# Eight heads' global scores in one block a batch, and eight value tiles a head instead of nine

## The reference, cut to what matters

```python
# 4 batches, 8 heads, 512 local and 32 global tokens, head size 64
k_all = concatenate([k_g, k_l]); v_all = concatenate([v_g, v_l])       # 544 keys
out_g = softmax(scale * q_g @ k_all.T) @ v_all                         # the 32 global queries see all
s_ll  = where(|i - j| <= 32, scale * q_l @ k_l.T, -1e9)                # local ones see a window of 32
out_l = softmax([scale * q_l @ k_g.T, s_ll]) @ v_all                   # and the global keys
x = [out_g, out_l] as 2304 tokens x 512
x = soft mixture of 8 experts (router phi, w1, relu, w2) of x
out = (h - tanh(h)) @ w_out,  h = x @ w_in
```

## Time and profile before

| | us |
|---|---|
| median of 3 runs (lowest, highest) | 318.64 (318.07, 319.13) |
| time of the profiled execution | 318.87 |
| its span | 317.1 |
| busy: PE, DVE, ACT, POOL | 306.9, 211.9, 139.0, 64.8 |

### The profile page before, as it was taken

How to read it: one execution, slowest core, us unless ns; L and a number is a source line. 1 busy time by engine, 2 the same in 40 slices (tenths; PEclk the granted TensorE clock), 3 DMA queues, 4 the chain that set the end, 5 groups by cost and what they waited for, 6 DMA issues and landing times.

```text
span 317.1 us, 7840 instructions
## 1 busy us (share of the span) xinstructions
PE 306.9 (97%) x2987; PEld 220.3 (69%) x2987; DVE 211.9 (67%) x443; ACT 139.0 (44%) x293; POOL 64.8 (20%) x62
## 2 busy tenths in 40 slices
PE   7999999999999999999998999999999999999994
PEld 4576777777777786233335888788888888888883
DVE  3887988888889556721258877566556666566572
ACT  1366766666566642111137554432334222532531
POOL 0543434434335001000008964000000000000000
PEclk9999999999999999999999999999999999999999
DMA  7999999999999969999999000030003000300202
GB/s 236 376 375 341 334 377 407 370 401 372 375 390 343 391 232 378 414 407 412 415 419 406 21 2 0 1 132 2 0 0 134 0 0 0 135 1 0 99 2 74
DMA packets 18032, 69.56 MB, mean 219 GB/s; under 512 B 4176, under 2 KB 5840, under 8 KB 14288
## 3 DMA queue, kind: packets, MB, share of 16 engines
q1 hardware_dynamic: 18000, 69.14, 57.7%
HBM read 64.41 MB, written 4.46 MB: 217 GB/s over the span
## 4 chain that ended last, share of the span: by engine, by line
PE 86%; DVE 7%; issue 5%; ACT 1%; POOL 1%; DVEq 0%; POOLq 0%
PE ps L846 20%; PE ps L849 20%; PE ps L550 6%; PE ps L595 5%; PE ps L821 5%; PE ps L746 4%; PE ps L777 4%; PE ps L587 3%; PE ps L566 3%; DVE sc L1101 3%; PE ps L606 2%; PE ps L541 2%; PE ps L560 2%; PE ps L581 2%; PE ps L658 1%
## 5 line engine op out<-in xcount | busy, mean ns | idle before, releaser
L849 PE MATMUL ps<-wlo,gg 128*128 128x512 f32 x204 | 80.5, 395 | 0.0
L846 PE MATMUL ps<-whi,gg 128*128 128x512 f32 x204 | 80.3, 394 | 0.0
L1307 DVE SCALAR_TENSOR_TENSOR nt<-uu,ps 128x512 f32<-128x512 f32 (+2 forms) x80 | 48.4, 607 | 47.3 <-ACT uu L1008 47.1
L1008 ACT ACTIVATE uu<-ps 128x512 f32<-128x512 f32 (+2 forms) x80 | 42.8, 537 | 84.0 <-PE ps L821 78.2
L457 POOL TENSOR_TENSOR sc<-sc,mx 128x640 f32<-128x640 f32 x32 | 40.1, 1253 | 53.5 <-DVE mx L1106 53.5
L1318 DVE TENSOR_TENSOR gg<-nt,ps 128x512 fp32r<-128x512 f32 (+2 forms) x80 | 47.9, 601 | 0.1
L846 PEld LDWEIGHTS ps<-whi,gg 128*128 128x128 f32 x204 | 38.4, 188 | 8.8
L849 PEld LDWEIGHTS ps<-wlo,gg 128*128 128x128 f32 x204 | 38.4, 188 | 8.0
L1101 DVE TENSOR_TENSOR sc<-ps,cst 128x640 f32<-128x640 f32 x32 | 26.2, 820 | 7.5 <-PE ps L550 5.9
L821 PE MATMUL ps<-cT,Pst 128*128 128x512 f32 (+2 forms) x80 | 28.9, 361 | 0.7 <-DVE Pst L1289 0.6
L595 PEld LDWEIGHTS ps<-vv,eT 128*64 128x64 f32 x512 | 18.7, 137 | 13.4 <-issue 11.0
(11 more groups left out here) (130 smaller groups left out, 384.6 us busy)
## 6 DMA issues: line engine op xcount, KB each, us to landing
w<-moe_w SPq DMA_DIRECT2D x11, 2048.0 KB, 11.2
vv<-v_t SPq DMA_DIRECT2D x8, 1170.0 KB, 7.7
w<-moe_w SPq DMA_DIRECT2D x14, 512.0 KB, 11.6
kT<-k_t SPq DMA_DIRECT2D x16, 416.0 KB, 6.3
out<-oo SPq DMA_DIRECT2D x17, 256.0 KB, 2.2
qT<-q_t SPq DMA_DIRECT2D x16, 256.0 KB, 7.3
win<-moe_w_in SPq DMA_DIRECT2D x4, 1024.0 KB, 16.6
wout<-moe_w_out SPq DMA_DIRECT2D x3, 1024.0 KB, 22.2
```

Of the source, the lines that this page charges most:

```text
L846: pe.matmul(o, g, hi, start=(c == 0), stop=False)
L849: mm = pe.matmul(o, g, lo, start=False, stop=(c == NC - 1))
L1008: nc.scalar.activation(uu[c % 2][:, 0:width], cols(h_bank(i, c), width), ACT.Square, scale=(1.0 / 3) ** 0.5).then_inc(square_ready, 1)
L1307: nc.vector.scalar_tensor_tensor(out=nt[c % 2][:, 0:width], in0=uu[c % 2][:, 0:width], scalar=1.0, in1=cols(h_bank(i, c), width), op0=ALU. ...
```

## The change

The scores of both global units of a batch are made in one block, `scores(4)`: eight matmuls of 512 keys, then two times four of 32 keys. Unit 4 uses banks 0 and 1, unit 9 banks 2 and 3. Head j of unit 9 puts its 32 queries at rows `32 * (j ^ 1)` instead of `32 * j`, so that heads j and j+4, which read the same 64 rows, write other columns. `SCORES_AT` loses unit 9, so at k=4 no scores are made. `rank` gives the new order of the score counters (0 to 4, 9, 5 to 8). DVE passes both global units after `normalise` of unit 9 (`global_maxima`) and nothing after that of unit 4; `scg` and `gmx` are there twice.

A global unit's last 32 keys are now transposed as the end of a block of 96 columns, so they land on rows 64 to 95 of `eT`, and are weighed with those rows of the last odd value tile, by matmuls of 32 rows, second in the order of the tiles. The fifth even tile is gone from the layout and from the loads (1040 KB a load instead of 1170).

The loads of the last two pairs' keys and of the global queries count on one semaphore, and they, and the queries, are issued in another order.

```diff
-        SCORES_AT = {(u - AHEAD) % U: u for u in (0, 2, 4, 5, 7, 9)}
+        SCORES_AT = {(u - AHEAD) % U: u for u in (0, 2, 4, 5, 7)}
+        GR = P // 2 + SG
+        def rank(k):
+            return k if k < 5 else 5 if k == 9 else k + 1
+        def global_rows(qd, j):
+            return 32 * (j ^ qd)
-            return 0 if k in GQ else 2 * head_of(k)[1]
+            return 2 * (k // 5) if k in GQ else 2 * head_of(k)[1]
...
             def keys(i, pr):
-                sp.wait_ge(scores_ready, U * (i - 1) + GQ[pr // 2] + 1)
+                sp.wait_ge(scores_ready, U * (i - 1) + (6, 6, 8, 10)[pr])
...
             global_queries(1)
+            keys(1, 2)
+            keys(1, 3)
             sp.wait_ge(zeros_ready, 2)
             values(1, 0)
-            keys(1, 2)
             queries(1, 2)
-            keys(1, 3)
             queries(1, 3)
...
                 queries(i + 1, 0)
                 queries(i + 1, 1)
+                global_queries(i + 1)
+                keys(i + 1, 2)
+                queries(i + 1, 2)
                 load_w1(sp, i - 1, w1_loaded, w1s[i - 1][:])
-                keys(i + 1, 2)
                 keys(i + 1, 3)
-                global_queries(i + 1)
+                queries(i + 1, 3)
                 values(i + 1, 0)
-                queries(i + 1, 2)
-                queries(i + 1, 3)
...
                 if k in GQ:
-                    pe.wait_ge(qg_loaded, 16 * i)
-                    pe.wait_ge(masked_ready, U * i + k - 1)
+                    pe.wait_ge(global_loaded, 48 * i)
                 else:
...
+                pe.wait_ge(masked_ready, U * i + rank(k))
...
+                    for j in range(4):
+                        for qd in range(2):
+                            one(qd, j, 0)
+                    for qd in range(2):
                         for j in range(4):
+                            mm = one(qd, j, 1)
+                        mm.then_inc(scores_ready, 1)
...
-                    pe.transpose(cols(5, P, odd)[0:SG, :], e[:, 512:544], ident).then_inc(gprobsT_ready, 1)
+                    pe.transpose(cols(5, P, odd)[0:GR, :], e[:, SL + SG - GR:SL + SG], ident).then_inc(gprobsT_ready, 1)
...
-                    for c in range(5):
-                        if c == 4:
+                    for c in (0, 4, 1, 2, 3):
+                        if c == 3:
                             waits()
                         for j in range(4):
+                            r = slice(GR - SG, GR) if c == 4 else slice(0, P)
+                            v = vo[qd][r, j ^ qd, 3, :] if c == 4 else ve[qd][:, j ^ qd, c, :]
...
+            def global_maxima(i):
+                for qd in range(2):
+                    k = GQ[qd]
+                    dve.wait_ge(scores_ready, U * i + rank(k) + 1)
+                    dve.wait_ge(probsT_ready, U * (i - 1) + k + 1)
+                    dve.sem_inc(passed_by_dve, 1)
                     nc.vector.tensor_tensor_reduce(
...
-                    if k + 5 < U:
+                    if k + 5 < U - 1:
                         maxima(i, k + 5)
-                    elif not last:
+                    elif k == U - 1 and not last:
+                        global_maxima(i + 1)
+                    elif k + 5 >= U and not last:
                         maxima(i + 1, k + 5 - U)
```

More of the change, by code:

```diff
@@ L120, in program @@
         eT = [place(f"eT{n}", [P, 640], F32) for n in range(2)]
-        scg = place("scg", [P, SL + SG], F32)
+        scg = [place(f"scg{n}", [P, SL + SG], F32) for n in range(2)]
         mx = [place(f"mx{n}", [P, 4], F32) for n in range(2)]
-        gmx = place("gmx", [P, 2], F32)
+        gmx = [place(f"gmx{n}", [P, 2], F32) for n in range(2)]
         den = place("den", [P, 4], F32)
@@ L247, in program @@
         zeros_ready, memsets_done, rowmax_ready, c_repeated = (sem(n) for n in ("zeros_ready", "memsets_done", "rowmax_ready", "c_repeated"))
-        qg_loaded = sem("qg_loaded")
-        qk_loaded = [sem(f"qk_loaded{n}") for n in range(4)]
+        global_loaded = sem("global_loaded")
+        qk_loaded = [sem(f"qk_loaded{n}") for n in range(2)]
+        q_loaded = {n: sem(f"q_loaded{n}") for n in (2, 3)}
         v_loaded = [sem(f"v_loaded{n}") for n in range(2)]
@@ L297, in probs_of @@
         def probs_of(k):
-            return scg if k in GQ else pr[k % 2]
+            return scg[k // 5] if k in GQ else pr[k % 2]
         def lowered(i, k):
@@ L530, in scores, with one @@
             def scores(k):
-                bank = scores_ps(k)
                 if k in GQ:
-                    for part in range(2):
-                        for j in range(4):
[L536 to L542, removed]
+                    def one(qd, j, part):
+                        pr = 2 * qd + j // 2
+                        r = slice(64 * (j % 2), 64 * (j % 2) + 64)
+                        own = kT[pr][r, 0:768].rearrange("r (b n) -> r b n", n=96)[:, :, 0:64]
+                        keys = kT[pr][r, 768:768 + SG] if part else own
+                        at = global_rows(qd, j)
+                        o = ps[at:at + 32, scores_ps(GQ[qd]) + part, 0:SG if part else 512]
+                        return pe.matmul(o, qgT[r, pr, :], keys, start=True, stop=True)
+                    for j in range(4):
+                        for qd in range(2):
+                            one(qd, j, 0)
+                    for qd in range(2):
+                        for j in range(4):
+                            mm = one(qd, j, 1)
+                        mm.then_inc(scores_ready, 1)
                 else:
@@ new lines, in global_maxima, with maxima @@
+                        scg[qd][:], cols(scores_ps(k), SL + SG), cst[:, C_ZERO:C_ZERO + 1].broadcast_to([P, SL + SG]),
+                        1.0, -3.0e38, ALU.add, ALU.max, gmx[qd][:, 0:1]).then_inc(masked_ready, 1)
+                for qd in range(2):
+                    dve.wait_ge(masked_ready, U * i + rank(GQ[qd]) + 1)
+                    nc.vector.tensor_scalar(gmx[qd][:, 1:2], gmx[qd][:, 0:1], -SCALE, None, ALU.mult).then_inc(gmax_ready, 1)
+            def maxima(i, k):
+                dve.wait_ge(scores_ready, U * i + rank(k) + 1)
+                h = head_of(k)[2]
+                dve.wait_ge(exp_ready, U * i + (unit_of(h - 2) if h >= 2 else unit_of(h + 6) - U) + 1)
+                bank = scores_ps(k)
+                nc.vector.tensor_tensor(sc[h % 2][:].rearrange("p (b n) -> p b n", b=2),
+                                        ps[:, bank:bank + 2, 0:320],
+                                        cst[:, C_MASK:C_MASK + 640].rearrange("p (b n) -> p b n", b=2),
+                                        ALU.add).then_inc(masked_ready, 1)
+                dve.wait_ge(masked_ready, U * i + rank(k) + 1)
+                nc.vector.tensor_reduce(mx[h % 2][:], sc[h % 2][:].rearrange("p (j n) -> p j n", j=4),
+                                        AX.X, ALU.max).then_inc(max_ready, 1)
@@ L1430, in attention_layout @@
     v = np.concatenate([v, np.zeros((NB, NH, P, D + 1), np.float32)], axis=2)
-    tiles = [v[:, :, P * c:P * c + P] for c in range(5)] + [v[:, :, 64 + P * c:64 + P * c + P] for c in range(4)]
-    v_t = np.stack(tiles, axis=2).reshape(NB, 2, 4, 9, P, D + 1).transpose(0, 1, 4, 2, 3, 5).reshape(NB, 2, P, -1)
+    tiles = [v[:, :, 64 * a + P * c:64 * a + P * c + P] for a in range(2) for c in range(4)]
+    v_t = np.stack(tiles, axis=2).reshape(NB, 2, 4, 8, P, D + 1).transpose(0, 1, 4, 2, 3, 5).reshape(NB, 2, P, -1)
     vg_t = with_one(v_g).reshape(NB, 2, 4, SG, D + 1).transpose(0, 1, 3, 2, 4)
```

57 lines of the change are left out of this document (19 added, 38 removed).

## The result

The kernel after takes 320.37 us (median of 15 executions, 319.56 to 321.32), the kernel before 319.12 (15 executions): 1.25 us more, a ratio of 1.0042 with a 95% interval of 1.003 to 1.0054. The profiled execution spans 318.5 us against 317.1. The prediction had 319.3 us, +0.62. Its largest chance, 0.51, went to a change of at most 0.96 us; by that limit the kernel is slower, which had 0.39. The time lies inside its range, the loss is twice what it summed up. Of the 1.07 us between 319.3 and 320.37, 0.48 come from the starting point: the kernel before was taken at 318.64 from three executions and has 319.12 in fifteen.

The account below looks back on a forecast made before the run. It took TensorE and VectorE, each nearly filling a 24.90 us batch, and their waits on each other as the bound. Start +1.54, three full batches +0.72 -1.00 each, then the end, gave +0.62 on 318.64: 319.3 us, range 317.8 to 321.3.

Parts of the forecast that it names:

- The block: Merged global scores block on PE: eight tiles run at once, 1.12 us, bounds 1.05 to 2.10.
- The two shape changes: Global unit's weighing on PE: going into and out of 32-row matmuls costs +0.24 us a unit, bounds 0 to 0.34.
- The gate: Before the merged block: it now waits for the mask of unit 3 and starts 0.70 us late.
- Half a batch later: At k=4: block gone -1.05, shape changes +0.24, the 0.19 us wait gone; together -1.00 us.
- The start: First batch: block waits for the next mask, starts at 15.12 instead of 13.53; scores 5 come +1.54 us.
- The last batch: End of batch 4: shift of +0.70 at scores 5 shrinks to +0.38 at turn 8.
- scores 5, +0.72: Full batch, after the merged block: next scores wait for both global passes and start at 67.33 against 66.61.
- level: Start of scores 5 in a full batch: VectorE's path gives 67.33, the PE path alone 67.30.
- (a): Merged block: eight tiles don't run at once, block 0.88 us longer; 322.4 to 322.8 us, chance 0.10.
- (b): Before the merged block: mask of unit 3 is no gate; 317.8 us, as low as 316.9, chance 0.12.
- (c): PE's waits dearer: 0.34 a unit, values 0.6 late, or clock falls before first block; 319.6 to 321.4, chance 0.25.
- The new order of the loads: At the start, last pairs' keys land first values some 2.2 us later; cost taken as 0, at most 0.6.

Follow-up runs that it names:

- run 3: Kernel after, with heads j and j+4 on the same 32 columns and same 64 rows, so sharing one array tile: 323.47 us, ratio 1.0137.
- run 1: Kernel before, with only the eight value tiles and the shape changes, its two global blocks kept: 320.48 us, ratio 1.0051.
- run 2: Kernel after, with a global unit's small product on all 128 rows, no shape change, global output rows wrong: 320.06 us, ratio 1.0028.
- run 11: Kernel before, its first global block also waiting for the mask of unit 3, with one extra 512-column product in that wait: 320.36 us, ratio 1.0046.
- run 4: Kernel after, with DVE masking unit 3 earlier, ahead of unit 8's normalisation and, before the first batch, unit 2's maximum: 319.91 us, ratio 1.003.
- run 5: Kernel of run 4, with DVE's two global passes ahead of the normalisation of unit 9, the small multiplications behind it: 319.09 us, ratio 1.0003.
- run 9: Kernel after, with one extra 512-column product, result thrown away, in TensorE's wait before the first block: 320.58 us, ratio 1.0049.
- run 7: Kernel before, with its first global block also waiting for the mask of unit 3: 321.27 us, ratio 1.0066.
- run 8: Kernel after, with the counter increment ahead of each global pass on DVE done twice: 320.95 us, ratio 1.0055.
- run 10: Kernel of run 6, with one extra 512-column product in the wait before the first block: 318.09 us, ratio 0.9972.
- run 6: Kernel of run 5, with the last 32 keys' rows in a zero-padded buffer of their own, so no shape change: 318.01 us, ratio 0.997.

## Why the prediction was right and wrong

**Right.** The block: 1.08 us for 1.12, eight tiles at once; run 3 shows that their being distinct is the cause. The Trainium skill's rule in "TensorEngine Tiling (Array Packing)", Gotcha 1 (PSUM Pressure), that different row tiles can't use one PSUM bank at the same time, does not hold in this trace: eight products of both row halves, each writing partitions of its own, ran in 0.45 us in two banks. The two shape changes: +0.27 us a unit for +0.24; run 1 shows it alone, and run 2 shows that it goes when the changes go. The Trainium skill's "TensorEngine Tiling (Array Packing)", Key Properties, says that changing the mode drains TensorE, and the trace agrees in that the two changes cost time, 0.27 us. The gate: the mask of unit 3 holds the block, 0.69 us late relative to the scores of units 0 and 1 (forecast 0.70). Half a batch later -0.97 for -1.00. The start: block at 15.09 for 15.12. The scores of units 2 and 3 came 0.34 us later in this execution (10.86 for 10.52), but the masks behind them did not (12.22 for 12.25, 13.82 for 13.85), since in the kernel before the first of them waited for ScalarE; so none of the +1.71 is that scatter. It is 0.17 over the forecast +1.54 by the term below. Run 11 has the late start at 1.3 us by itself. The last batch gave back 0.46 us, forecast 0.32.

**Wrong: the term "scores 5, +0.72" of a full batch.** It is +0.96. The prediction let the first pass start when "the block's first four heads are done", 1.13 us after the block's start. That is the length it gave to the whole block, 1.12 us, so the time from TensorE's last product to VectorE's start was put at next to nothing, without a reason. In the code the 512-column products of the two halves alternate, so the first half is done hardly before the second, and the pass starts 0.37 us after the block's end: 1.45 us. A hint stood in the rows of before: the mask at 80.58 starts 0.21 us after its scores, which end at 80.37. The two passes then took 1.38 us, not the 1.46 summed, so the scores come 3.15 us after the block where the prediction had 2.90. The working called DVE's path and PE's "level"; in truth DVE's is longer, and PE's last weighing ahead of the scores shows it as a stall, 1.01 us for 0.69. With +0.96 and -0.97, a batch gains nothing, instead of 0.28 us; only the first gains 0.30, as its wait of 0.26 us at 29.03 goes. Three full batches were to take the shift from 1.54 to 0.70 us, and took it from 1.71 to 1.40. That is 0.53 us of the 0.56 between forecast and measured shift; the start (+0.17, the same term in the first batch) and the last batch (-0.14) nearly cancel. Runs 4 and 5 bear this out: where DVE masks and passes sooner, the same TensorE work takes 24.48 to 24.50 us a batch, with PE idle for 0.37 us and not 0.60, and the median falls by 1.3 us, with the shift at the start still in it. The window of the fifth kernel from block to block:

```profile
64.42:88.90 24.48, 24.11 (x440) 1.00 1.01 381
```

**What the loss is made of.** The late start is 1.3 us (run 11), the shape changes 1.2 us (run 1: 0.30 us in each of four batches), and against these 2.5 us the merged block gives 0.31 us a batch (24.90 us with it and the shape changes, 25.21 with the changes alone), 1.2 us in four. The sum, +1.3, fits the 1.25 measured, closer than its terms are known: the intervals of runs 1 and 11 span 1.2 and 0.9 us. The table above splits the profile's shift in another way: 1.71 us late after the start, 0.30 back in the first batch, 0.01 in the next two, 0.46 back in the last and 0.24 more for its second weighing: 1.18. On TensorE the block that went was 1.05 us a batch. Of that, 0.31 reaches the period; the rest went to the gate ahead of the merged block and to the later passes behind it. How much each took cannot be added up from the runs: run 4 shows that when the first goes, the second grows.

**The rivals.** (a) fell, by run 3 and the rows of the block. (b) fell: the mask is the gate, run 4 moves it and the block follows. (c), dearer waits, with 319.6 to 321.4 us, is the case whose time came, though mostly not by its causes: the shapes cost 0.27 and not 0.34 us, no values were late, and what was dearer is the way from the block to the passes on DVE. That the time fell into its range by another mechanism is luck. Its falling clock did come, in four of fifteen executions of the kernel after, and is worth some 0.14 us of the median (run 9). The new order of the loads was tested by no run alone; up to 130 us PE waited for no DMA after the start, before or after.

## What to carry to other kernels

When two blocks are merged into one, their consumers are merged as well: follow the first consumer from the end of the merged block, not from where the half of the work would have been done, and ask what stands before it in its engine's order. A small product that adds no columns to TensorE's work can still cost two changes of tile shape, here 0.27 us; zero rows in a buffer of their own avoid them. A wait moved into the first pass of a pipelined loop is paid there in full, whatever the later passes make of it.

## What the runs showed of the hardware

- The granted clock fell in some executions only: a mean clock of 0.991 to 0.995 stands in four of the fifteen of the kernel after, in five of eight of run 2 and in three of twelve of run 5, and in none of the kernel before. Behind waits of 1.73 and 1.91 us before the first block, the profiles of runs 7 and 8 have 0.56 and 0.50 from 17 to 19 us, that of the kernel after has 1.00 there, behind a wait of 1.91 us too. With one product of 0.95 us in the wait it stayed at 1.00 in the profiles of runs 9 to 11.
- The start scatters. TensorE's scores of units 2 and 3 started anywhere from 10.28 to 11.50 us in the profiled executions, of kernels that issue the same transfers up to there, each time some 0.46 us after the mask of unit 1 had ended (10.06 and 10.52 in the kernel before, 10.40 and 10.86 in the kernel after). Most of it comes from the first scores block, 1.32 us long in the kernel before, 1.64 in the kernel after and 2.28 in run 5:

```profile
6.12 1.32 PE L550 MATMUL ps<-kT,qT 64*64 64x160 f32 x32
6.12 2.28 PE L564 MATMUL ps<-kT,qT 64*64 64x160 f32 x32
```

Its matmuls have records of up to 0.53 us there, for 0.30 us; the granted clock reads 1.00, and no run shows the cause. In runs 4 and 8 the first mask waited for a DMA of constants instead. The first global block mostly follows this start, so a single profile can't tell shifts of the start below a microsecond.
- A second scatter: a piece of the weights of the last layers (`win`). In the kernel after and in runs 2, 7, 8, 10 and 11 PE waited for it. The line is that of the kernel after; the kernel before had no wait there:

```profile
168.51 1.06 PE L891 MATMUL ps<-win,soT 128*32 128x512 f32 x8 [0.64 <-DMA win<-moe_w_in]
```

It adds 0.2 us to the distance between the two profiles (1.18 to 1.4). Runs 7 and 11, which are the kernel before but for its start, have it, and runs 3, 4, 5, 6 and 9, with the merged block, do not, so no cause in the change is shown.
